# An attention-with-decay kernel: the state product leaves the natural-order y and is added to the turned y

## The chip, the cores and the metric

The kernel runs on one core of one Trainium2 chip. The metric is the device time of one execution in microseconds (us). The kernel before took 431.91 us, the median of three runs (431.82 to 432.13).

## The reference

Three layers follow one another. The first is a linear attention whose state decays, for 4 batches, 8 heads, 768 positions and a head width of 48:

```python
for t in range(S):
    kt, vt, rt, wt = (k[:, :, t], v[:, :, t], r[:, :, t], w[:, :, t])
    cur = np.einsum('bhd,bhe->bhde', u[None] * kt, vt)
    y[:, :, t] = np.einsum('bhd,bhde->bhe', rt, state + cur)
    state = wt[:, :, :, None] * state + np.einsum('bhd,bhe->bhde', kt, vt)
```

Its output, 3072 tokens of 384 values, goes through `g = h * clip(h + 3, 0, 6) / 6` with `h = x @ w_in` (384 by 2048) and `g @ w_out`, and then through a soft mixture of 8 experts with 4 slots each (`phi`, `w1`, `w2`).

## The kernel before

The attention is computed in 24 units: 4 batches times 6 chunks of 128 positions, unit n being batch n % 4 of chunk n // 4. A unit handles 8 heads as 4 pairs; a pair's two heads lie on partitions 0 to 47 and 64 to 111, so an operand that holds a pair has 112 partitions. Inside a chunk the decays are running products along the positions (two scans on VectorE, L817 and L829), keys and receptances are multiplied by them on GpSimd (L1341, L1350), and then:

- `score` (L445): keys times receptances, one 128 by 128 product for each head, two heads at once on the two halves of the array's rows; VectorE masks the result (L843), ScalarE and GpSimd split it into two half-precision parts.
- `attend` (L502): y in natural order (128 positions by 384 values) in one PSUM bank, `y_ps`. For each pair one f32 product of the decayed receptances (stationary, 112 by 128) with the state of the chunks before (moving, 112 by 96, L510), then, on top of it, six f16 products of the split scores with the split values (L516 to L520, 48 columns each). Units 0 to 3 have no state and go through `attend_first`.
- `finish_y` (L862, VectorE) scales y, adds the diagonal term and writes `y_nat`; `turn_x` (L527, TensorE) transposes it in three pieces of 128 columns back into `y_ps`; ScalarE and VectorE split the turned y into the operand of the next layer (`high_x` L1152, `low_x` L877).
- `increment` (L470): keys (transposed by `turn_keys`, L454) times values, 64 and 48 rows of output at a time; VectorE adds it to the state (`add_state`, L872, two instructions); the state of unit n is decayed by GpSimd (`decay_state`, L1359).

The second layer runs through all of this. Its 96 steps (6 groups of 512 tokens, 16 steps each) are `mlp(s)`: nine f16 products of 512 columns (L544 to L546) into one of two PSUM banks, then a relu on ScalarE (L1184), a gate and a 32 by 32 transposition on VectorE (L904, L914). `mlp(s)` waits for the gate of step s - 2. Four steps belong to one unit and are called its phases. The order on each engine is written out by hand: TensorE does the scores of unit n in phase 0, the turning of unit n - 1 at the start of phase 1 ahead of `mlp(s)` (only for the first unit behind it), the keys of unit n in phase 2 ahead of `mlp(s)` and its increment behind it, and `attend(n)` behind `mlp(s)` in phase 3. From step 5 of a group on, and in the next group, `add_logits` (L579) takes four steps' gates at a time as 32-row products, and at the turn of a group `fold_logits` (L586), `natural_logits` (L591) and `gather_slots` (L611) follow; a chain of maximum, exponential and sums on VectorE and ScalarE belongs to them. Waits are on semaphores and each engine works in order.

The part behind step 96 (from about 330 us on) is the mixture of experts.

Of the kernel before, what the change touches and what calls it, by code (L numbers as in the profile page):

```python
# [6 lines left out]
ACT = mybir.ActivationFunctionType  # L7
# [4 lines left out]
P = 128  # L12
# [8 lines left out]
Y_SCALE = V_SCALE * SCORE_SCALE  # L21
# [3 lines left out]
B, H, S, D = 4, 8, 768, 48  # L25
# [3 lines left out]
PB = H // 2  # L29
# [3 lines left out]
PD = ALIGN + D  # L33
# [10 lines left out]
W_PIECES = 8  # L44
WP = KT * FF // W_PIECES
LAST_INC = UNITS - B


def build_program(nc, wT, rkT, nat_in_dram, u, u_blocks, w_in, w_outT, w_out, phi, w1, w2, out):
    with ExitStack() as ctx:  # L50
# [21 lines left out]
        r_dec = [carve(PB * P) for _ in range(2)]  # L72
# [3 lines left out]
        scores_hi, scores_lo = (t.bitcast(F16) for t in rk_prod)  # L76
        k_nat = carve(PB * PD)
        v_hi = [carve(DM // 2).bitcast(F16) for _ in range(2)]
# [4 lines left out]
        y_nat = carve(DM)  # L83
        state = [pairs(carve(PB * 2 * D), 2 * D) for _ in range(B)]
# [12 lines left out]
        ident = sb("ident", P)  # L97
# [100 lines left out]
        k_ps = ctx.enter_context(nc.psum_tensor("k_ps", [P, 512], F32))  # L198
        inc_ps = ctx.enter_context(nc.psum_tensor("inc_ps", [P, 512], F32))
        y_ps = ctx.enter_context(nc.psum_tensor("y_ps", [P, 512], F32))  # L200
# [41 lines left out]
        decayed = sem("decayed")  # L242
# [6 lines left out]
        k_nat_done = sem("k_nat_done")  # L249
        inc_ready = sem("inc_ready")  # L250
        y_ready = sem("y_ready")
# [14 lines left out]
        x_turned = sem("x_turned")  # L266
# [65 lines left out]
        def is_unit(n):  # L332
            return 0 <= n < UNITS
# [99 lines left out]
        def _(pe):  # L433
# [66 lines left out]
                last.then_inc(y_ready, 1)  # L500

            def attend(n):  # L502
                b = n % B
                pe.wait_ge(x_lo_done, n)
                pe.wait_ge(decayed, n - B + 1)
                pe.wait_ge(v_lo_done, n - B + 1)
                pe.wait_ge(scores_lo_done, n - B + 1)
                for p in range(PB):
                    both = y_ps[:, p * 2 * D:(p + 1) * 2 * D]
                    pe.matmul(both, r_dec[n % 2][0:PD, p * P:(p + 1) * P], state[b][0:PD, p, :],  # L510
                              start=True, stop=False, skip_group_check=True)
                    for j in range(2):
                        c = both[:, j * D:(j + 1) * D]
                        here = slice((j * PB + p) * P, (j * PB + p + 1) * P)
                        there = slice((2 * p + j) * D, (2 * p + j + 1) * D)
                        pe.matmul(c, scores_hi[:, here], v_hi[n % 2][:, there], start=False, stop=False,  # L516
                                  skip_group_check=True)
                        pe.matmul(c, scores_hi[:, here], v_lo[n % 2][:, there], start=False, stop=False,
                                  skip_group_check=True)
                        last = pe.matmul(c, scores_lo[:, here], v_hi[n % 2][:, there], start=False, stop=True,  # L520
                                         skip_group_check=True)
                last.then_inc(y_ready, 1)

            def turn_x(n):
                pe.wait_ge(y_done, n + 1)
                for q in range(KT):
                    last = pe.transpose(y_ps[:, q * P:(q + 1) * P], y_nat[:, q * P:(q + 1) * P], ident[:])  # L527
                last.then_inc(x_turned, 1)

            def mlp(s):  # L530
                g, i = divmod(s, FT)
# [112 lines left out]
            for s in range(END):  # L644
                n, phase = unit_of(s)
# [164 lines left out]
        def _(dve):  # L810
# [29 lines left out]
            def mask_scores(n):  # L840
                dve.wait_ge(scores_ready, 2 * n + 2)
                dve.wait_ge(scores_lo_done, n - B)
                nc.vector.tensor_tensor(scores.rearrange("p (o n) -> p o n", o=PB),  # L843
                                        sc_ps[:, :].rearrange("p (o n) -> p o n", o=PB),
                                        mask[:].rearrange("p (o n) -> p o n", o=1).broadcast_to([P, PB, 2 * P]),
                                        ALU.mult).then_inc(masked, 2)
# [18 lines left out]

            def add_state(n):
                dve.wait_ge(inc_ready, 2 * n + 2)
                for j in range(2):
                    rows = slice(ALIGN * j, ALIGN * j + D)
                    s = state[n % B][rows, :, j * D:(j + 1) * D]  # L870
                    new = pairs(inc_ps[rows, 0:PB * 2 * D], 2 * D)[:, :, j * D:(j + 1) * D]
                    last = nc.vector.tensor_tensor(s, s, new, ALU.add)  # L872
                last.then_inc(state_added, 1)
# [137 lines left out]
            for s in range(END):  # L1011
                n, phase = unit_of(s)
                g, i = divmod(s, FT)
                if s <= 1:
                    gate(s)
                    turn_gated(s)
                if phase == 0:
                    if is_unit(n - 1):
                        finish_y(n - 1)
                    if n - 1 < LAST_INC:  # L1020
                        add_state(n - 1)
                if phase == 1:
                    if is_unit(n):
                        mask_scores(n)
                    if is_unit(n + 1):
                        scan_suffix(n + 1)
                        restart_prefix(n + 1)
                    if is_unit(n - 1) and n % B == 0 and n > B:
                        low_x(n - 1)
                    if g >= 1 and i == 2:  # L1030
                        group_maximum(g - 1)
                if phase == 2:
                    if g >= 1 and i == 3:
                        turn_weight(g - 1)
                        sum_weight(g - 1)
                    if is_unit(n - 1) and n % B:
                        low_x(n - 1)
                    if is_unit(n):
                        sum_diag(n)
                        low_v(n)  # L1040
                if s == 0:
                    low_w(1)
                    sum_diag(B)
                if phase == 3:
                    if is_unit(n + 1):
                        scan_prefix(n + 1)
                    if s == STEPS + 4:
                        dve.wait_ge(run_sum_done, C)
                        nc.vector.tensor_scalar(run_sum, run_sum, 1e-9, None, ALU.add).then_inc(sum_inv_step, 1)
                        dve.wait_ge(sum_inv_step, 1)  # L1050
                        nc.vector.reciprocal(run_sum, run_sum).then_inc(sum_inv_step, 1)
                        dve.wait_ge(sum_inv_step, 2)
                        nc.vector.tensor_scalar(fold_inv[:], fold32, run_sum, None, ALU.mult).then_inc(fold_inv_done, 1)
                        dve.wait_ge(fold_inv_done, 1)
                        nc.vector.tensor_scalar(fold_alpha, fold_inv[:], alpha, None, ALU.mult).then_inc(fold_inv_done, 1)
                    if 1 <= g < C and i == 4:
                        add_slots(g - 1)
                if s == 4:
                    dve.wait_ge(w_phi_ready, 4)
                    nc.vector.transpose(w_phi[:], l_ps[:]).then_inc(w_phi_done, 1)  # L1060
                if s == STEPS - 12:
                    cols, tiles = c_parts[0]
                    dve.wait_ge(logits_done, C - 1)
                    nc.vector.tensor_reduce(cmax[:, tiles], by_slot(soft[:, cols]), AX_X, ALU.max).then_inc(c_max_done, 1)
                if s == STEPS - 8:
                    c_inverse(0)
                if s == STEPS:
                    copy_cT(1)
                    copy_cT(0)
                if 1 < s < STEPS:  # L1070
                    gate(s)
                    turn_gated(s)
# [46 lines left out]
        def _(act):  # L1119
# [22 lines left out]
            def copy_keys(n):  # L1142
                act.wait_ge(k_turned, n + 1)
                if n:
                    act.wait_ge(inc_ready, 2 * n)
                nc.scalar.activation(k_nat, k_ps[:, 0:PB * PD], ACT.Copy, scale=Y_SCALE).then_inc(k_nat_done, 1)

            def high_x(n):
                act.wait_ge(x_turned, n + 1)
# [87 lines left out]
            for s in range(END):  # L1237
                n, phase = unit_of(s)
# [57 lines left out]
        def _(pool):  # L1296
# [46 lines left out]
            def decay_receptance(n):  # L1343
                pool.wait_ge(prefix_done, n + 1)
                pool.wait_ge(rk_rows_in[n % B], 16 * (n // B + 1))
                if n >= 2:
                    pool.wait_ge(scores_ready, 2 * (n - 1))
                    pool.wait_ge(y_ready, n - 1)
                dst, receptance, decay = receptance_of(n)
                nc.gpsimd.tensor_tensor(dst, receptance, decay, ALU.mult).then_inc(r_dec_done, 1)  # L1350

# [135 lines left out]
```

## Time and profile before

| | |
|---|---|
| median of three runs | 431.91 us |
| the profiled execution's own time | 432.12 us |
| its span, first to last instruction | 430.4 us |
| TensorE busy | 410.6 us, 95% |
| VectorE busy | 333.8 us, 78% |
| ScalarE, GpSimd busy | 155.4 us, 196.4 us |
| mean granted TensorE clock | 0.992 of 2.4 GHz |

The profile is of one execution. A share of busy time is a mean over the whole span, so it says which engine to look at and not what a change is worth. Ends of matmuls are modelled and successive matmuls overlap, so what one matmul costs is read from the distance between starts, not from its own length. An f32 product shows as two records with the same line, an f16 product as one.

### The profile page before, as it was taken

The numbers are of one execution on the slowest core, as the hardware profiler recorded it, in microseconds if no ns is written. First come the engines' busy times: TensorE is split into PE (matmuls) and PEld (weight loads), VectorE is DVE, ScalarE is ACT, GpSimd is POOL, SyncE is SP. The second block draws the span as 40 slices with busy tenths as digits, with TensorE's granted clock in tenths as the row PEclk, the third lists the DMA queues.
The fourth block names the chain that finished last, engine by engine and source line by source line (L and its number), as shares of the span: only waits on it lengthen the run. The fifth ranks groups of instructions, "written<-read, shape, count | busy, mean of one in ns | idle before, by whom it ended". The sixth has DMA issues, their size and how long they took to land.

```text
span 430.4 us, 9672 instructions
## 1 busy us (share of the span) xinstructions
PE 410.6 (95%) x3898; PEld 222.6 (52%) x3898; DVE 333.8 (78%) x535; ACT 155.4 (36%) x263; POOL 196.4 (46%) x183
## 2 busy tenths in 40 slices
PE   8999899999999999999999999989999999999981
PEld 3875555556555555555565555455554443433430
DVE  7798799998988989889889889898866687641142
ACT  2265355533334244144342342432333234211142
POOL 7747888874645663455654456634630012010000
PEclk9999999999999999999999999999999999999996
DMA  8996312468034223403440332131008961589829
GB/s 248 354 392 250 121 60 63 121 244 283 17 111 121 72 55 116 123 0 121 121 121 2 121 119 86 44 113 56 2 0 339 404 216 70 225 319 423 354 83 357
DMA packets 15245, 69.35 MB, mean 161 GB/s; under 512 B 2016, under 2 KB 2656, under 8 KB 13152
## 3 DMA queue, kind: packets, MB, share of 16 engines
q1 hardware_dynamic: 15200, 68.73, 45.0%
q8 instruction: 31, 0.51, 0.5%
q14 instruction: 14, 0.11, 0.1%
HBM read 64.00 MB, written 4.72 MB: 160 GB/s over the span
## 4 chain that ended last, share of the span: by engine, by line
PE 74%; DVE 8%; issue 6%; DMA 5%; POOL 3%; ACT 2%; SPq 0%; POOLq 0%; DVEq 0%
PE hid L544 13%; PE hid L546 12%; PE hid L545 12%; PE l_ps L579 5%; PE y_ps L510 5%; PE l_ps L611 4%; PE sc_ps L445 4%; DMA att<-rkT_dram 3%; PE hid L757 2%; PE inc_ps L470 2%; PE y_ps L527 2%; DVE att L817 2%; PE sc_ps L611 1%; PE hid L738 1%; PE sc_ps L738 1%
## 5 line engine op out<-in xcount | busy, mean ns | idle before, releaser
L1184 ACT ACTIVATE relu<-hid,three 128x512 f32<-128x512 f32 x96 | 65.9, 687 | 141.7 <-PE hid L546 140.9
L544 PE MATMUL hid<-x_split,w_split 128*128 128x512 f16 x288 | 109.4, 380 | 0.0
L546 PE MATMUL hid<-x_split,w_split 128*128 128x512 f16 x288 | 109.1, 379 | 0.0
L545 PE MATMUL hid<-x_split,w_split 128*128 128x512 f16 x288 | 109.1, 379 | 0.0
L904 DVE SCALAR_TENSOR_TENSOR gated<-relu,hid 128x512 f32<-128x512 f32 x96 | 65.1, 679 | 28.3 <-ACT relu L1184 27.7
L914 DVE STREAM_TRANSPOSE ring<-gated 128x512 f32<-128x512 f32 x96 | 68.3, 711 | 3.3
L1332 POOL TENSOR_TENSOR att<-att 128x1024 f16<-128x1024 f32 x20 | 40.5, 2026 | 50.6 <-ACT att L1129 50.6
L1350 POOL TENSOR_TENSOR att<-att 112x512 f32<-112x512 f32 x19 | 22.4, 1181 | 58.7 <-DVE att L829 58.7
L544 PEld LDWEIGHTS hid<-x_split,w_split 128*128 128x128 f16 x288 | 28.2, 98 | 37.5 <-issue 8.6
L546 PEld LDWEIGHTS hid<-x_split,w_split 128*128 128x128 f16 x288 | 28.1, 98 | 34.0
L545 PEld LDWEIGHTS hid<-x_split,w_split 128*128 128x128 f16 x288 | 28.2, 98 | 25.1 <-issue 0.3
L510 PE MATMUL y_ps<-att 112*128 112x96 f32 x160 | 33.7, 295 | 1.1 <-DVE att L888 1.1
L1341 POOL TENSOR_TENSOR att<-att 112x512 f32<-112x512 f32 x22 | 27.9, 1266 | 8.2 <-DVE att L817 6.5
L445 PEld LDWEIGHTS sc_ps<-att 48*128 48x128 f32 x384 | 23.4, 187 | 12.6 <-issue 11.8
L817 DVE TENSOR_TENSOR_SCAN att<-att 112x517 f32<-112x517 f32 x22 | 28.1, 1278 | 1.5 <-DMA att<-wT_dram 1.5
L445 PE MATMUL sc_ps<-att 48*128 48x128 f32 x384 | 27.9, 284 | 1.4 <-issue 1.1
L510 PEld LDWEIGHTS y_ps<-att 112*128 112x128 f32 x160 | 24.9, 189 | 5.5 <-issue 3.7
L611 PE MATMUL l_ps<-ring,soft 32*32 32x512 f32 x192 | 25.5, 594 | 1.8 <-DVE soft L936 1.8
L1152 ACT ACTIVATE x_split<-y_ps 128x384 f16<-128x384 f32 x24 | 11.8, 490 | 42.8 <-PE y_ps L527 42.8
L829 DVE TENSOR_TENSOR_SCAN att<-att 112x517 f32<-112x517 f32 x22 | 27.2, 1235 | 0.0
L611 PE MATMUL sc_ps<-ring,soft 32*32 32x512 f32 x384 | 26.1, 598 | 0.0
L579 PE MATMUL l_ps<-gated,w_phi 128*32 128x512 f32 x192 | 25.6, 605 | 0.4 <-DVE gated L904 0.4
(228 smaller groups left out, 752.5 us busy)
## 6 DMA issues: line engine op xcount, KB each, us to landing
att<-nat_dram SPq DMA_DIRECT2D x20, 576.0 KB, 4.1
att<-rkT_dram SPq DMA_DIRECT2D x22, 448.0 KB, 5.5
att<-w_dram SPq DMA_DIRECT2D x5, 1536.0 KB, 14.2
att<-wT_dram SPq DMA_DIRECT2D x22, 226.2 KB, 4.8
out_dram<-w_split SPq DMA_DIRECT2D x12, 384.0 KB, 3.9
stage<-w_in_dram SPq DMA_DIRECT2D x2, 1536.0 KB, 13.5
ring<-w_outT_dram SPq DMA_DIRECT2D x1, 3072.0 KB, 15.7
stage<-w_dram SPq DMA_DIRECT2D x2, 1536.0 KB, 9.9
```

The lines of the kernel that those rows point to most:

```text
L445: last = pe.matmul(sc_bank[j][:, cols], k_dec[n % 2][rows, cols], r_dec[n % 2][rows, cols], start=True, stop=True)
L510: pe.matmul(both, r_dec[n % 2][0:PD, p * P:(p + 1) * P], state[b][0:PD, p, :], start=True, stop=False, skip_group_check=True)
L544: pe.matmul(hid[s % 2][:], high, x_high, start=(q == 0), stop=False)
L545: pe.matmul(hid[s % 2][:], high, x_low, start=False, stop=False)
L546: last = pe.matmul(hid[s % 2][:], low, x_high, start=False, stop=(q == KT - 1))
L579: pe.matmul(l_ps[SLOTS * c:SLOTS * (c + 1), :], w_phi[:, i * SLOTS:(i + 1) * SLOTS], gated_tile(g * FT + i), start=(m == 0), stop=(m == 3) ...
L611: ins = pe.matmul(dg_bank[a][SLOTS * c:SLOTS * (c + 1), :], weight_T[SLOTS * a:SLOTS * (a + 1), b * SLOTS:(b + 1) * SLOTS], ring_group(g, ...
L817: nc.vector.tensor_tensor_scan(suffix[0:PD, ::-1], w_rows_of(n)[0:PD, ::-1], mark[0:PD, ::-1], 1.0, ALU.mult, ALU.add).then_inc(suffix_don ...
L904: nc.vector.scalar_tensor_tensor(gated_tile(s), relu_tile(s), 6.0 * GATE, hid[s % 2][:], ALU.min, ALU.mult).then_inc(gated_done, 1)
L914: nc.vector.transpose(ring_tile(s), gated_tile(s)).then_inc(gated_turned, 1)
L1184: nc.scalar.activation(relu_tile(s), hid[s % 2][:], ACT.Relu, bias=three[:], scale=GATE / H_SCALE)\
L1332: nc.gpsimd.tensor_tensor(scores_lo, scores, scores_hi, ALU.subtract).then_inc(scores_lo_done, 1)
```

## The change

The state product leaves `attend`, whose first score product now starts the accumulation. In `turn_x` the three transpositions put the turned y into `y_ps`, and eight f32 products are then added on top of it in the same bank: the state is the stationary operand, 64 or 32 of its 96 columns at a time, and the receptances of a pair stream as 128 columns. The eight pieces are cut so that each lies in one 128-row block of the turned y and starts at a multiple of its own height. Both operations are part of the same signal `x_turned`.

What follows from it elsewhere: the state is not scaled any more, so `copy_keys` loses its scale; `add_state(n)` also waits for the turned y of unit n and moves from phase 0 of VectorE to phase 1, behind the mask (for unit 4 to phase 2); the receptances of unit n wait for the turned y of unit n - 2 where they waited for its natural y; `attend` does not wait for the decayed state, the product in `turn_x` does.

```diff
+STATE_ROWS = ((0, 64), (64, 32), (96, 32), (128, 64), (192, 64), (256, 32), (288, 32), (320, 64))
...
             def attend(n):
-                b = n % B
                 pe.wait_ge(x_lo_done, n)
-                pe.wait_ge(decayed, n - B + 1)
                 pe.wait_ge(v_lo_done, n - B + 1)
                 pe.wait_ge(scores_lo_done, n - B + 1)
                 for p in range(PB):
                     both = y_ps[:, p * 2 * D:(p + 1) * 2 * D]
-                    pe.matmul(both, r_dec[n % 2][0:PD, p * P:(p + 1) * P], state[b][0:PD, p, :],
-                              start=True, stop=False, skip_group_check=True)
...
             def turn_x(n):
                 pe.wait_ge(y_done, n + 1)
                 for q in range(KT):
-                    last = pe.transpose(y_ps[:, q * P:(q + 1) * P], y_nat[:, q * P:(q + 1) * P], ident[:])
+                    last = pe.matmul(y_ps[:, q * P:(q + 1) * P], y_nat[:, q * P:(q + 1) * P], ident[:], start=(q == 0),
+                                     stop=True, is_transpose=True, skip_group_check=True)
+                if n >= B:
+                    last = add_state_product(n)
                 last.then_inc(x_turned, 1)
+
+            def add_state_product(n):
+                pe.wait_ge(decayed, n - B + 1)
+                for first, size in STATE_ROWS:
+                    q, row = divmod(first, P)
+                    p, col = divmod(first, 2 * D)
+                    last = pe.matmul(y_ps[row:row + size, q * P:(q + 1) * P], state[n % B][0:PD, p, col:col + size],
+                                     r_dec[n % 2][0:PD, p * P:(p + 1) * P], start=False, stop=True,
+                                     skip_group_check=True)
+                return last
...
             def add_state(n):
                 dve.wait_ge(inc_ready, 2 * n + 2)
+                dve.wait_ge(x_turned, n + 1)
...
                 if phase == 0:
                     if is_unit(n - 1):
                         finish_y(n - 1)
-                    if n - 1 < LAST_INC:
-                        add_state(n - 1)
                 if phase == 1:
                     if is_unit(n):
                         mask_scores(n)
+                    if B < n - 1 < LAST_INC:
+                        add_state(n - 1)
...
                 if phase == 2:
+                    if n == B + 1:
+                        add_state(B)
...
-                nc.scalar.activation(k_nat, k_ps[:, 0:PB * PD], ACT.Copy, scale=Y_SCALE).then_inc(k_nat_done, 1)
+                nc.scalar.activation(k_nat, k_ps[:, 0:PB * PD], ACT.Copy).then_inc(k_nat_done, 1)
...
-                    pool.wait_ge(y_ready, n - 1)
+                    pool.wait_ge(x_turned, n - 1)
```

On TensorE, around the turning of unit 8 at the end of the first group (L445 are scores, L527 the transpositions, L544 to L546 an `mlp` step), the order before is:

```order
L586 MATMUL l_ps<-soft,fold 128x512
L445 MATMUL sc_ps<-att 128x128 x8
L527 MATMUL y_ps<-ident,att 128x128 x3
L544 MATMUL hid<-x_split,w_split 128x512
L545 MATMUL hid<-x_split,w_split 128x512
L546 MATMUL hid<-x_split,w_split 128x512
```

In the changed kernel the same place reads as follows (L524 are the transpositions, L535 the state products, L554 to L556 the `mlp` step):

```order
L596 MATMUL l_ps<-soft,fold 128x512
L446 MATMUL sc_ps<-att 128x128 x8
L524 MATMUL y_ps<-ident,att 128x128 x3
L535 MATMUL y_ps<-att 64x128
L535 MATMUL y_ps<-att 32x128 x2
L535 MATMUL y_ps<-att 64x128 x2
L535 MATMUL y_ps<-att 32x128 x2
L535 MATMUL y_ps<-att 64x128
L554 MATMUL hid<-x_split,w_split 128x512
```

Eight products with 64, 32, 32, 64, 64, 32, 32 and 64 rows of output now stand between the last transposition and the `mlp` step; the four products of 96 columns are gone from `attend`, which stands one `mlp` step ahead of these rows.

On VectorE, in the same two phases, the order before is (L862 finishes y, L872 adds to the state, L904 and L914 are gate and transposition, L843 is the mask, L817 and L822 begin the next unit's decays, L921 is the group's maximum):

```order
L862 SCALAR_TENSOR_TENSOR att<-y_ps,att 128x384
L872 TENSOR_TENSOR att<-att,inc_ps 48x4x48 x2
L904 SCALAR_TENSOR_TENSOR gated<-relu,hid 128x512
L914 STREAM_TRANSPOSE ring<-gated 128x512
L843 TENSOR_TENSOR att<-sc_ps,mask 128x1024
L817 SCALAR_TENSOR_TENSOR att<-att 112x517
L822 RECIPROCAL att<-att 112x4
L921 TENSOR_REDUCE stats<-l_ps 128x1
```

And in the changed kernel (L872, L883, L915, L925, L853, L827, L832 and L932 are the same instructions):

```order
L872 SCALAR_TENSOR_TENSOR att<-y_ps,att 128x384
L915 SCALAR_TENSOR_TENSOR gated<-relu,hid 128x512
L925 STREAM_TRANSPOSE ring<-gated 128x512
L853 TENSOR_TENSOR att<-sc_ps,mask 128x1024
L883 TENSOR_TENSOR att<-att,inc_ps 48x4x48 x2
L827 SCALAR_TENSOR_TENSOR att<-att 112x517
L832 RECIPROCAL att<-att 112x4
L932 TENSOR_REDUCE stats<-l_ps 128x1
```

The two additions to the state have moved from ahead of a gate to between the mask and the scan.

## Rows read from the trace of the kernel before

**Rows 1.** The page: TensorE's share, granted clock by slices, last chain.

```profile
PE 410.6 (95%) x3898; PEld 222.6 (52%) x3898; DVE 333.8 (78%) x535; ACT 155.4 (36%) x263; POOL 196.4 (46%) x183
...
PEclk9999999999999999999999999999999999999996
...
PE 74%; DVE 8%; issue 6%; DMA 5%; POOL 3%; ACT 2%; SPq 0%; POOLq 0%; DVEq 0%
```

**Rows 2.** Groups by line, TensorE: shapes, count | busy us, mean ns | idle before.

```profile
L510 PE MATMUL y_ps<-att 112*128 112x96 f32 x160 | 33.7, 295 | 1.1 <-DVE att L888 1.1
```

**Rows 3.** Timeline of TensorE, one `attend`: start us, length us, instruction, count.

```profile
189.28 0.38 PE L546 MATMUL hid<-x_split,w_split 128*128 128x512 f16 x1
189.49 0.36 PE L510 MATMUL y_ps<-att 112*128 112x96 f32 x2
189.69 0.19 PE L516 MATMUL y_ps<-att 128*128 128x48 f16 x1
...
189.82 0.18 PE L520 MATMUL y_ps<-att 128*128 128x48 f16 x1
189.84 0.44 PE L510 MATMUL y_ps<-att 112*128 112x96 f32 x2
...
191.14 0.38 PE L544 MATMUL hid<-x_split,w_split 128*128 128x512 f16 x1
```

**Rows 4.** Timeline of TensorE, one `increment`: whole, its third and its last record.

```profile
186.63 0.38 PE L546 MATMUL hid<-x_split,w_split 128*128 128x512 f16 x1
186.94 0.67 PE L470 MATMUL inc_ps<-att 128*64 128x48 f32 x16
...
187.04 0.22 PE L470 MATMUL inc_ps<-att 128*64 128x48 f32 x1
...
187.39 0.22 PE L470 MATMUL inc_ps<-att 128*64 128x48 f32 x1
187.54 0.39 PE L544 MATMUL hid<-x_split,w_split 128*128 128x512 f16 x1
```

**Rows 5.** Timeline of TensorE: scores, logits, turning, with single records inside.

```profile
193.18 1.16 PE L445 MATMUL sc_ps<-att 48*128 48x128 f32 x16
...
193.39 0.27 PE L445 MATMUL sc_ps<-att 48*128 48x128 f32 x1
...
194.07 0.27 PE L445 MATMUL sc_ps<-att 48*128 48x128 f32 x1
194.27 0.64 PE L579 MATMUL l_ps<-gated,w_phi 128*32 128x512 f32 x4
...
194.72 0.61 PE L579 MATMUL l_ps<-gated,w_phi 128*32 128x512 f32 x4
195.26 0.55 PE L527 MATMUL y_ps<-ident,att 128*128 128x128 f32 x3
195.65 0.38 PE L544 MATMUL hid<-x_split,w_split 128*128 128x512 f16 x1
```

**Rows 6.** Timeline at the turn of a group, VectorE, and TensorE's next `mlp` step.

```profile
160.21 0.71 DVE L872 TENSOR_TENSOR att<-att,inc_ps 48x192 f32<-48x192 f32 x2
162.00 0.69 DVE L904 SCALAR_TENSOR_TENSOR gated<-relu,hid 128x512 f32<-128x512 f32 x1 [1.08 <-ACT relu L1184]
...
163.36 1.19 DVE L843 TENSOR_TENSOR att<-sc_ps,mask 128x1024 f32<-128x1024 f32 x1
164.47 1.22 DVE L817 TENSOR_TENSOR_SCAN att<-att 112x517 f32<-112x517 f32 x1
...
163.51 0.38 PE L544 MATMUL hid<-x_split,w_split 128*128 128x512 f16 x1
```

**Rows 7.** Timeline of TensorE: three matmuls ahead of which it waited.

```profile
70.91 0.32 PE L510 MATMUL y_ps<-att 112*128 112x96 f32 x1 [0.53 <-DVE att L888]
...
169.48 0.26 PE L470 MATMUL inc_ps<-att 128*64 128x48 f32 x2 [0.69 <-ACT att L1146]
...
47.57 0.38 PE L445 MATMUL sc_ps<-att 48*128 48x128 f32 x2 [1.08 <-issue]
```

More of the change, by code:

```diff
@@ L515, in attend @@
                         there = slice((2 * p + j) * D, (2 * p + j + 1) * D)
-                        pe.matmul(c, scores_hi[:, here], v_hi[n % 2][:, there], start=False, stop=False,
+                        pe.matmul(c, scores_hi[:, here], v_hi[n % 2][:, there], start=True, stop=False,
                                   skip_group_check=True)
```

## Prediction

> **What bounds the kernel now.** I began with the page. TensorE is busy for 410.6 of 430.4 us and makes up 74% of the chain that ended last; the granted clock stands in its upper tenth in every slice but the last [rows 1]. A busy TensorE can still have slack, so the second view was its timeline over one unit. There the matmuls follow each other start to start without a hole: after the last `mlp` matmul at 189.28 the first of `attend` starts at 189.49, the same 0.21 us that one `mlp` matmul of 512 columns takes [rows 3]. The third view was where TensorE did wait. It waits in few places: ahead of `attend` for the low half of the values (0.53 us in unit 6, the same again in unit 7), at three turns of a group for the chain behind the group's maximum (0.69 us ahead of the increment in the row shown), and once, at 47.57, ahead of the scores of unit 5 (1.08 us) [rows 7]. So up to the end of the units the time is the sum of TensorE's spacings, and what the change adds or takes between two starts passes into the total, apart from these few places.
>
> **What goes.** Units 4 to 23, which are 20, have a state product: 160 records of L510 are 20 units by 4 pairs by 2 [rows 2]. One `attend` takes 1.65 us, from its first start at 189.49 to the next `mlp` step at 191.14 [rows 3]. Six score products of a pair lie between 189.69 and 189.84, which is 0.155 us for six or 0.026 each, so the 24 that remain take 0.62 us. The change takes 1.65 - 0.62 = 1.03 us out of a unit. In unit 4 that gives nothing: the scores of unit 5 stand behind it and wait 1.08 us anyway [rows 7], for receptances that GpSimd is still decaying. So 19 x 1.03 = 19.6 us.
>
> **What comes.** Sixteen records (eight f32 products) behind the transpositions. The trace has no product of this kind, so I build it from three prices.
>
> First, the stream. The scores are f32 with 128 moving columns as well: from 193.39 to 194.07 six records of one half of the array start, 0.11 us apart, while the other half runs beside them [rows 5]. Two records of a product on one place of the array therefore take 0.22 us. Products on different columns of the array do run at the same time: the four 32-column products of the logits all start at 194.27 and their second records at 194.72, 0.45 us later, although each streams 512 columns [rows 5]. Were there no such overlap, the eight would take 8 x 0.22 = 1.76 us; with perfect overlap the three that share a place take 0.66.
>
> Second, the first load of weights, which nothing hides: in the increment the second record of a place comes 0.10 us after the first and the rest every 0.06 ((187.39 - 187.04) / 6) [rows 4], so 0.04 more for 64 columns; for 32 columns it is 0.45 - 0.43 = 0.02 [rows 5].
>
> Third, the price of a change of shape. Wherever two neighbours use the array with different tile shapes, the next start is late: 186.63 to 186.94 is 0.31 where 0.21 is the stream (full array to 64 columns); 187.39 to 187.54 is 0.15 where 0.06 is (64 columns to full); 194.07 to 194.27 is 0.20 where 0.11 is (half rows to 32 columns); 194.72 to 195.26 is 0.54 where 0.43 is (32 columns to full) [rows 4, 5]. That is 0.09 to 0.11 each time, whatever the pair; I take 0.095. Where the shape stays (112 rows of 128 columns behind an `mlp` matmul, the transpositions ahead of one) nothing is added [rows 3, 5].
>
> The sequence is 64 | 32 32 | 64 64 | 32 32 | 64 rows of output: five stretches, with four changes of height inside and one at either end. What no row shows is a change between 64 and 32 columns. Its price lies between nothing, if pieces on different columns don't care about each other's height, and 0.095 us with all of the stretch before it drained. I take 0.095, since every change of shape that the trace has costs that, also the ones in which the number of rows stays at 128 and only the columns change. Then a 64-row stretch takes 0.22 + 0.04 = 0.26, a 32-row stretch 0.24, and the block 3 x 0.26 + 2 x 0.24 + 6 x 0.095 = 1.83 us. 20 units give 36.6 us.
>
> The Trainium skill speaks on both sides here. "TensorEngine Tiling (Array Packing)", Performance Considerations, recommends just this swap with column tiles where the moving operand is narrow, with up to a twofold gain; its Key Properties say that a change of the tiling mode, as opposed to a change of tile, drains the engine, and list 128 by 64 and 128 by 32 as two modes. By the second rule the sum above stands; by the first alone the block would be 0.89 us. The trace agrees with the drain on every pair it has (0.09 to 0.11 us); the pair 64 and 32 no row shows.
>
> **What the waits give back.** The waits of units 6 and 7 stand behind a chain on VectorE. It now holds the two additions to the state as well (0.71 us [rows 6]), but TensorE arrives 1.83 us later, so both waits of 0.53 us [rows 7] go: -1.1 us. At the three turns VectorE's chain from the mask to the exponential sets the wait for the keys. Before, the scan began at 164.47, 0.96 us after the `mlp` step at 163.51 [rows 6]. Now VectorE waits for the turned y, which comes at about the start of that step, adds 0.71 and scans some 0.8 behind it: 0.1 us earlier relative to TensorE, -0.3 us over the three. In phase 0 the additions lay in front of a gate that had 1.08 us of idle time [rows 6], so taking them away there gives nothing. In phase 1 their cover is the longer turning itself. GpSimd's new wait is for a turning two units back, and ScalarE's copy without a scale is the same instruction; both cost nothing. ScalarE's split of the turned y and of the scores comes later by as much as TensorE does, and `attend` is two steps away.
>
> **Sum.** +36.6 - 19.6 - 1.1 - 0.3 = +15.6 us on the profiled execution's 432.12 us, which is 447.7. The runs' median lies 0.2 below that execution: 447.5 us. With the three prices moved by their rounding (0.08 to 0.11 for a change, 0.02 to 0.06 for a first load) this case alone gives 444 to 451.
>
> **Rivals.**
>
> Free heights, on the other side: a 32-row piece starts while a 64-row piece on other columns runs, and nothing drains inside the block. What speaks for it is that the increments' 64 and 48 columns run side by side and even overtake each other; against it, that both sit in tiles of the same height. Then the places work as queues of three products: 0.04 + 6 x 0.11 + 2 x 0.095 = 0.89 us, 17.8 for 20 units, against 19.6 gone and some 0.6 less waiting: -2.4, or 429.5 us. It decides for faster from a block below about 1.0 us.
>
> A drain by place only: a piece waits for the pieces of another height on its own columns, not for all. Each column then sees one change inside: 0.04 + 0.44 + 0.095 + 0.02 + 0.22 + 0.19 = 1.01 us, 20.2 in all, less 19.6 and 0.6: nothing, or 431.9 us, no change. For it: array columns are served separately. Against it: the same drains.
>
> The wait on VectorE takes over: with a short block the mask (1.19 us) ends after the turning, the additions are no longer covered and push the chain at three turns and in units 6 and 7 by 0.71 us: up to +3.6 on the case of free heights, 433.1. Against it: the mask starts at 163.36 and ends 0.15 us behind the step's start even then.
>
> No overlap inside a stretch: 8 x 0.25 + 0.57 = 2.57 us, 51.4 for 20 units, less 19.6 and 1.4: 462 us. The logits' rows speak against it.
>
> **Chances.** Drain at each change of height 0.70, free heights 0.16, drain by place 0.08, VectorE 0.04, no overlap 0.02. The likeliest case gives the time, 447.5 us. The range goes from the free heights, 429, to the top of the likeliest, 451. A measurement of this kernel can tell 0.2% (0.9 us) from no change: faster 0.17, within it 0.09, slower 0.74.
>
> **What would show it.** In the profile after: from the first transposition to the next `mlp` matmul 2.2 us (0.39 before) if each change drains, 1.3 if heights are free, 1.4 if by place. Inside, the 64-row and the 32-row records start in five stretches with 0.2 us between the last start of one and the first of the next, or interleaved if they are free. `attend` takes 0.62 us. The waits ahead of `attend` in units 6 and 7 are gone. I am wrong if the 32-row products start while the first 64-row product still streams.

## The result, and the profile after

The changed kernel takes 448.71 us, the median of four runs (447.99 to 449.84), the kernel before beside it 432.02 us (431.82 to 432.14, four runs): a ratio of 1.0387, with a 95% interval of 1.0375 to 1.0399. It is slower, by 16.7 us; the forecast was 447.5 us.

The page of the changed kernel answers to [rows 1]:

```profile
PE 427.8 (96%) x4058; PEld 217.8 (49%) x4058; DVE 331.6 (74%) x535; ACT 153.9 (34%) x263; POOL 199.9 (45%) x183
...
PEclk9999899999999999999999999999999999999996
...
PE 84%; DMA 5%; DVE 4%; issue 3%; ACT 1%; POOL 1%; SPq 0%; DVEq 0%; POOLq 0%
```

TensorE is busy for 17.2 us more, its share of the last chain has grown from 74 to 84%, and one slice of the granted clock has an 8. This profile is of the run of 449.37 us.

The block in question, by the starts of its records (timeline of TensorE: start us, length us, instruction, count):

```profile
204.29 0.55 PE L524 MATMUL y_ps<-ident,att 128*128 128x128 f32 x3
...
204.77 0.43 PE L535 MATMUL y_ps<-att 112*64 112x128 f32 x2
...
204.93 0.27 PE L535 MATMUL y_ps<-att 112*64 112x128 f32 x1
...
205.13 0.41 PE L535 MATMUL y_ps<-att 112*32 112x128 f32 x4
...
205.47 0.44 PE L535 MATMUL y_ps<-att 112*64 112x128 f32 x4
...
205.84 0.41 PE L535 MATMUL y_ps<-att 112*32 112x128 f32 x4
...
206.19 0.43 PE L535 MATMUL y_ps<-att 112*64 112x128 f32 x2
206.55 0.39 PE L554 MATMUL hid<-x_split,w_split 128*128 128x512 f16 x1
```

Five stretches, 0.34 to 0.37 us apart. Within the third the two 64-row products run side by side (four records in the time of two), so the array is shared inside a stretch and not between stretches. The clearest is the second stretch: its 32-row products write rows 64 to 127, on columns of the array that the first product leaves free, and still do not start beside it. The first product's second record starts at 204.93 and the next stretch 0.20 us behind it, where 0.11 is the stream of one record [rows 5]. From the first transposition to the `mlp` step it is 2.26 us, where it was 0.39 [rows 5]: 1.87 more.

`attend` answers to [rows 3]: without the four state products it is 0.61 us long (0.61 in 15 of the 20 units, 0.70 in the others).

```profile
74.68 0.38 PE L556 MATMUL hid<-x_split,w_split 128*128 128x512 f16 x1
74.89 0.19 PE L513 MATMUL y_ps<-att 128*128 128x48 f16 x1
...
75.47 0.18 PE L517 MATMUL y_ps<-att 128*128 128x48 f16 x1
75.50 0.38 PE L554 MATMUL hid<-x_split,w_split 128*128 128x512 f16 x1
```

I gave each matmul the distance to the next start, set idle time of more than 0.15 us apart, and summed by function over both traces. That is a ledger of the whole execution; the rows that did not change are left out:

| us, TensorE | before | after | difference |
|---|---|---|---|
| the eight state products in the turning | 0.0 | 35.6 | +35.6 |
| `turn_x` itself (one change of shape more) | 9.6 | 11.4 | +1.8 |
| `attend` | 34.0 | 12.6 | -21.4 |
| `mlp` and `score`, same instructions | 217.3 | 218.9 | +1.6 |
| waits ahead of scores | 1.4 | 3.8 | +2.4 |
| waits ahead of the gathering of slots | 1.8 | 0.4 | -1.5 |
| waits ahead of `attend` | 1.1 | 0.0 | -1.1 |
| waits ahead of the increment | 1.4 | 1.6 | +0.2 |

With -0.4 for the matmuls at the very start it is +17.2 us, and the profiled execution of after took 449.37 us against 432.12, 17.25 more.

The row of `mlp` and `score` is not work but the clock: in the run below that keeps the full clock the two come to 217.3 us again. The waits that answer to [rows 7]: units 6 and 7 no longer wait ahead of `attend`, the wait at the turn of a group has gone from 0.69 to 0.43 us, but unit 5's scores wait 2.21 us where they waited 1.08, and behind that wait the granted clock falls (timeline, then two tables by stretch, after and before: start and end, its length, then busy time and count of PE, PEld (TensorE's weight loads), DVE, ACT and POOL, granted clock, DMA share, GB/s):

```profile
47.22 0.42 PE L446 MATMUL sc_ps<-att 48*128 48x128 f32 x2 [2.21 <-issue]
...
178.71 0.26 PE L471 MATMUL inc_ps<-att 128*64 128x48 f32 x2 [0.43 <-ACT att L1159]
```

```profile
44.00:47.20 3.20, 1.01 (x9) 0.11 (x9) 3.09 (x5) 0.00 (x0) 2.90 (x3) 1.00 0.14 24
47.20:49.10 1.90, 1.88 (x17) 1.68 (x18) 0.00 (x0) 0.00 (x0) 1.82 (x3) 0.56 0.78 270
49.10:51.90 2.80, 2.80 (x11) 1.15 (x11) 2.67 (x2) 0.00 (x0) 2.44 (x2) 0.69 0.79 253
```

```profile
44.00:47.50 3.50, 2.49 (x39) 1.54 (x36) 3.47 (x7) 0.06 (x1) 2.86 (x3) 1.00 0.10 19
47.50:49.10 1.60, 1.53 (x18) 1.21 (x19) 0.85 (x3) 0.00 (x0) 1.60 (x2) 1.00 0.78 276
49.10:51.90 2.80, 2.80 (x19) 1.14 (x17) 2.47 (x3) 0.76 (x2) 2.72 (x3) 1.00 0.90 270
```

TensorE was busy for 1.01 of 3.20 us, and then works 3.4 us at 1.2 instead of 2.4 GHz (a mean of 0.56 over 1.90 and of 0.69 over 2.80 us). Before, the same place was busy for 2.49 of 3.50 us and stayed at full clock. The four runs stand at 448.0, 448.1, 449.4 and 449.8 us, those below with a mean clock of 0.992, those above with 0.982 and 0.988. Only the run of 449.37 us was profiled, and the mean clock of a run does not by itself tell where it fell: the kernel before has means from 0.985 to 0.994 among runs within 0.5 us of each other.

### The profile page after: what moved, and what is told of

The parts are those of the page before. It is cut to its first block, busy times and chain, and to the rows that moved or that the text cites. A ratio compares the mean times of both kernels' runs of the same rounds, so it can differ in the third digit from the quotient of the medians.

```text
span 447.7 us, 9988 instructions
## 1 busy us (share of the span) xinstructions
PE 427.8 (96%) x4058; PEld 217.8 (49%) x4058; DVE 331.6 (74%) x535; ACT 153.9 (34%) x263; POOL 199.9 (45%) x183
## 4 chain that ended last, share of the span: by engine, by line
PE 84%; DMA 5%; DVE 4%; issue 3%; ACT 1%; POOL 1%; SPq 0%; DVEq 0%; POOLq 0%
PE hid L554 14%; PE hid L556 13%; PE hid L555 13%; PE y_ps L535 8%; PE l_ps L589 5%; PE sc_ps L446 5%; PE l_ps L621 4%; DMA att<-rkT_dram 3%; PE inc_ps L471 2%; PE hid L767 2%; PE y_ps L524 2%; PE sc_ps L621 1%; PE k_ps L455 1%; PE l_ps L596 1%; PE hid L748 1%
## 5 line engine op out<-in xcount | busy, mean ns | idle before, releaser
L554 PE MATMUL hid<-x_split,w_split 128*128 128x512 f16 x288 | 110.1, 382 | 0.0
L556 PE MATMUL hid<-x_split,w_split 128*128 128x512 f16 x288 | 109.4, 380 | 0.0
L915 DVE SCALAR_TENSOR_TENSOR gated<-relu,hid 128x512 f32<-128x512 f32 x96 | 65.0, 677 | 30.8 <-ACT relu L1197 30.8
L1345 POOL TENSOR_TENSOR att<-att 128x1024 f16<-128x1024 f32 x20 | 45.0, 2252 | 62.2 <-ACT att L1142 62.2
L925 DVE STREAM_TRANSPOSE ring<-gated 128x512 f32<-128x512 f32 x96 | 68.3, 711 | 3.3
L554 PEld LDWEIGHTS hid<-x_split,w_split 128*128 128x128 f16 x288 | 28.2, 98 | 41.0 <-issue 11.5
L556 PEld LDWEIGHTS hid<-x_split,w_split 128*128 128x128 f16 x288 | 28.2, 98 | 34.4 <-issue 0.6
L535 PE MATMUL y_ps<-att 112*64 112x128 f32 (+1 forms) x320 | 37.0, 291 | 0.0
L827 DVE TENSOR_TENSOR_SCAN att<-att 112x517 f32<-112x517 f32 x22 | 28.1, 1278 | 1.6 <-DMA att<-wT_dram 1.2
L535 PEld LDWEIGHTS y_ps<-att 112*64 112x64 f32 (+1 forms) x320 | 17.4, 121 | 18.1 <-issue 18.1
## 6 DMA issues: line engine op xcount, KB each, us to landing
att<-rkT_dram SPq DMA_DIRECT2D x22, 448.0 KB, 5.4
```

The source lines that it names most:

```text
L535: last = pe.matmul(y_ps[row:row + size, q * P:(q + 1) * P], state[n % B][0:PD, p, col:col + size], r_dec[n % 2][0:PD, p * P:(p + 1) * P], ...
L554: pe.matmul(hid[s % 2][:], high, x_high, start=(q == 0), stop=False)
L556: last = pe.matmul(hid[s % 2][:], low, x_high, start=False, stop=(q == KT - 1))
L827: nc.vector.tensor_tensor_scan(suffix[0:PD, ::-1], w_rows_of(n)[0:PD, ::-1], mark[0:PD, ::-1], 1.0, ALU.mult, ALU.add).then_inc(suffix_don ...
L915: nc.vector.scalar_tensor_tensor(gated_tile(s), relu_tile(s), 6.0 * GATE, hid[s % 2][:], ALU.min, ALU.mult).then_inc(gated_done, 1)
L925: nc.vector.transpose(ring_tile(s), gated_tile(s)).then_inc(gated_turned, 1)
```

## The experiments

**The order of the heights.** Theory A: each change of height drains the array and costs some 0.095 us plus the overlap that it breaks. Theory B: the eight products simply cost what they stream, since 8 x 0.22 = 1.76 us is close to the measured 1.78. Only the order of the pieces changes:

```diff
-STATE_ROWS = ((0, 64), (64, 32), (96, 32), (128, 64), (192, 64), (256, 32), (288, 32), (320, 64))
+STATE_ROWS = ((0, 64), (192, 64), (128, 64), (320, 64), (64, 32), (96, 32), (256, 32), (288, 32))
```

> The same eight products in another order: the four of 64 rows first (alternating between the two halves of the columns), then the four of 32 rows. Theory A (every change of height drains the array): one change inside instead of four. From the changed kernel's starts the block is 0.09 to come in, 0.16 + 3 x 0.107 + 0.10 for the 64s and 0.36 for the 32s, 1.03 us where it was 1.87: 0.84 less for each of 20 units, some 16.8 us less, about 432 us. Theory B (the eight products cost what they stream, 8 x 0.22 one after the other): no change of the block, 448 us.

Measured: 433.56 us (433.19 to 433.79, four runs; before 432.01). The block, from the first transposition to the `mlp` step, is 1.43 us, 1.04 more than the transpositions alone. That is as expected. The time is 1.5 us above the 432 expected, and TensorE's waits are longer, 12.2 us in all where the kernel before has 9.0. The block's lines:

```profile
195.82 0.55 PE L524 MATMUL y_ps<-ident,att 128*128 128x128 f32 x3
196.30 1.02 PE L535 MATMUL y_ps<-att 112*64 112x128 f32 x16
197.25 0.39 PE L554 MATMUL hid<-x_split,w_split 128*128 128x512 f16 x1
```

The other way round, with as many changes as eight pieces allow:

```diff
+STATE_ROWS = ((0, 64), (64, 32), (128, 64), (96, 32), (192, 64), (256, 32), (320, 64), (288, 32))
```

> The same eight products with the heights alternating, 64, 32, 64, 32 and so on: seven changes inside instead of four, and no two products side by side. Theory A: four stretches of 0.363 and four of 0.335 and 0.09 to come in, 2.88 us for the block where it was 1.87, 20 us more: about 468 us. Theory B: the same streams, no change, 448 us.

Measured: 470.01 us (one run).

```profile
214.77 0.55 PE L524 MATMUL y_ps<-ident,att 128*128 128x128 f32 x3
215.25 2.86 PE L535 MATMUL y_ps<-att 112*64 112x128 f32 x16
218.04 0.39 PE L554 MATMUL hid<-x_split,w_split 128*128 128x512 f16 x1
```

3.27 us, 2.88 beyond the transpositions. The same eight products cost 1.04, 1.87 or 2.88 us by their order alone, with one, four and seven changes of height inside. B has fallen. The run is 2 us above the 468 expected; 1.6 of them are the granted clock, which falls behind unit 5's wait in this profile too (0.81 from 47.2 to 49.1 us and 0.52 from there to 51.9).

**One height.** Twelve products of 32 rows, 50% more of them, and no change inside.

```diff
+STATE_ROWS = tuple((32 * i, 32) for i in range(12))
```

> Twelve products of 32 rows instead of eight of 64 and 32, so no change of height inside the block at all; four columns of the array, three products on each. Theory A (drain at each change of height): 0.09 + 0.13 + 5 x 0.107 + 0.12 = 0.88 us for the block where it was 1.87, 20 us less: about 428 us, and that is less than the kernel before, since the block then costs less than the 1.04 us which attend lost. Theory B (the products cost what they stream, one after the other): twelve times 0.22, 2.6 us for the block, 15 us more, 464 us.

```profile
195.05 0.87 PE L535 MATMUL y_ps<-att 112*32 112x128 f32 x24
195.85 0.39 PE L554 MATMUL hid<-x_split,w_split 128*128 128x512 f16 x1
```

The block is 0.80 us from its first start to the `mlp` step and with the change of shape ahead of it 0.89, as expected. The time is not: 434.21 us (430.5 to 438.67, twelve runs; before 432.01), where I had 428. Two things are in it. TensorE now waits 5.6 us ahead of scores (1.4 before), and the runs spread over 8 us; the profiled one of them (433.02 us) stops for 1.7 us in the middle of the last gathering of slots, in front of an instruction that the profile shows waiting for nothing:

```profile
381.30 0.62 PE L621 MATMUL k_ps<-ring,soft 32*32 32x512 f32 x3 [1.71 <-issue]
```

**No state product.** The eight products are left out, so units 4 to 23 lack what the earlier chunks contribute; everything else is the changed kernel.

```diff
-                if n >= B:
-                    last = add_state_product(n)
```

> The state product is left out altogether (units 4 to 23 get no contribution of earlier chunks); all else is the changed kernel. Theory A (the time up to the last unit is the sum of TensorE's spacings): the block of 1.87 us goes 20 times, 37.5 us less, 411 us, plus what TensorE then waits. Theory C (VectorE's chain, with the additions to the state now between mask and scan, becomes the bound where the longer turning no longer covers it): waits of up to 0.7 us at several units and turns of a group, 414 us or more.

Measured: 422.06 us (one run), not 411. The products do go from TensorE (37.4 us), and 11 us come back as waits: 9.1 us ahead of scores (3.8 in the changed kernel), 3.7 ahead of increments (1.6), 2.2 ahead of the gathering (0.4), 1.2 ahead of `attend` and 0.7 ahead of `mlp`. The timeline at one of them:

```profile
141.46 1.19 DVE L837 TENSOR_TENSOR_SCAN att<-att 112x517 f32<-112x517 f32 x1
...
142.73 1.18 POOL L1361 TENSOR_TENSOR att<-att 112x512 f32<-112x512 f32 x1 [2.96 <-DVE att L837]
...
144.01 0.38 PE L446 MATMUL sc_ps<-att 48*128 48x128 f32 x2 [0.74 <-issue]
```

VectorE's second scan ends at 142.65, GpSimd decays the receptances until 143.91, and the scores start 0.1 us later. Theory A for this run holds for the work and not for the time: some 10 us below the kernel before, the chain of scan, receptances and scores is what TensorE waits for most, ahead of ten units' scores. C named VectorE's chain and 414 us or more, and the chain does begin at VectorE's scan; whether the additions to the state are what makes the scan late, no run shows.

**The clock at unit 5.** Six matmuls without use go into the longer wait.

```diff
                         attend(B)
                         weigh_phi(1)
+                        pe.wait_ge(masked, 2 * n)
+                        stay_warm(6, sc_bank[0])
```

> The changed kernel, and six f16 matmuls of 512 columns without use in the 2.2 us that TensorE waits for the receptances of unit 5, behind the waits for the masks and ahead of that for the receptances. Theory D (where the changed kernel takes 449.4 to 449.8 us and not 448.0, the granted clock fell after this longer wait): every run near 448.0 us, and the profile shows the full clock from 47 to 52 us. Rival (the spread comes from somewhere else, the weights' transfers or the code): the runs keep both times.

Measured: 448.17 us (447.8 to 448.5, four runs). The same stretches as above:

```profile
44.00:47.20 3.20, 2.47 (x18) 0.66 (x14) 3.15 (x5) 0.00 (x0) 2.85 (x3) 1.00 0.16 22
47.20:49.10 1.90, 1.83 (x20) 1.38 (x21) 0.56 (x1) 0.00 (x0) 1.82 (x3) 1.00 0.76 265
49.10:51.90 2.80, 2.80 (x22) 1.43 (x22) 2.17 (x3) 0.00 (x0) 2.80 (x2) 1.00 0.86 259
```

The clock stays full, `mlp` and `score` take 217.3 us again instead of 218.9, and no run comes near 449.4. So the fall of the clock cost the profiled run of the changed kernel 1.6 us. That the run of 449.84 had the same fall fits, but it was not profiled.

**Twelve products and the six matmuls.**

> The twelve products of 32 rows, and the six matmuls in the wait ahead of the scores of unit 5. Theory D: the runs above 430.5 us go for the part that is the clock at unit 5, the median at 431 us or below. Rival (the spread of 430.5 to 438.7 us comes from the stop of 1.7 us inside the last gathering of slots and the like, late in the kernel): it stays, median 434 us.

Measured: 433.21 us (430.5 to 436.33, twelve runs). Four runs stand at 430.5 to 430.8, eight at 433 to 436. So the clock at unit 5 was not what spreads this kernel; the rival stands. The profile of the twelve products alone agrees: its scores of unit 5 waited 2.21 us, and the granted clock stayed at 1.00 from 40 to 52 us.

**The scan moved.** In addition VectorE's second scan goes from the start of phase 3 to the end of phase 2.

```diff
+                if phase == 2 and is_unit(n + 1) or s == 0:
+                    scan_prefix(n + 1)
                 if phase == 3:
-                    if is_unit(n + 1):
-                        scan_prefix(n + 1)
```

> As the run before, and VectorE's second scan (of the decays for the receptances of the next unit) moved from the start of phase 3 to the end of phase 2, ahead of a gate for which ScalarE is still at work. Theory E (what the shorter attention does not give back is waited ahead of the scores, for the receptances that GpSimd decays after this scan): the waits ahead of the scores of units 6, 7 and 23 (0.86, 0.83 and 0.94 us) go, 2 to 2.5 us less than without the move. Rival (the scores wait for the keys or for the masks, or VectorE's gates come later by as much): no change or slower.

Measured: 433.29 us (432.91 to 437.45, twelve runs); its fastest run is 2.4 us above the fastest without the move. The waits ahead of scores did go, from 4.2 to 0.8 us, so theory E has the chain right (the units are 7, 8 and 23; the expectation counts the first two one too low). But the gates come later and `mlp` waits 3.9 us, which was nothing before, as the rival has it. Ahead of the scores of unit 7 without the move, and ahead of an `mlp` step of unit 6 with it:

```profile
74.95 0.38 PE L446 MATMUL sc_ps<-att 48*128 48x128 f32 x2 [0.84 <-issue]
```

```profile
74.22 0.39 PE L554 MATMUL hid<-x_split,w_split 128*128 128x512 f16 x1 [1.07 <-DVE gated L917]
```

> The kernel before with the same move of the scan and nothing else. Theory E: its scores wait in one place only (unit 5), which the move does not touch, so no change, 432 us, within 0.5 us.

Measured: 432.77 us (432.56 to 433.21, ten runs; before 432.03), a ratio of 1.0012 with an interval of 0.9993 to 1.0031. The medians are 0.7 us apart, outside the 0.5 us that I expected, and all ten runs lie above all but two of the 29 of before, one of which stood at 436.72 us and widens the interval. Here too `mlp` gets a wait (1.6 us in all) that it did not have, while the 1.1 us ahead of `attend` go.

**Where the code's pieces end.** The profile's queue of instructions moves packets of 16 KB, 33 of them in the run with twelve products (31 before); I take them for TensorE's code, since their number goes with its matmuls (31 at 3898, 34 at 4294). In the run that stopped, one of them was fetched at 378.9 us, 3.8 us after the last gathering's first matmul; in the profiled run with the six matmuls, which did not stop, the same one was fetched 0.3 us ahead of it. To move the ends of the pieces without other work, the first ten matmuls without use are cut smaller (40 of 128 columns, then 80 of 64):

```diff
-            keep_awake(10)
+            keep_awake(40, 128)
```

> As the twelve products of 32 rows with the six matmuls in unit 5's wait, and TensorE's first ten matmuls without use (512 columns, ahead of the first scores) cut into forty of 128 columns: the same streaming, some 60 instructions more. Theory F (half of the runs of the kernel with twelve products stand at 433 to 436 us and not at 430.5 because a piece of TensorE's code is fetched late inside the last gathering of slots, as the profile of its first version shows with a stop of 1.7 us; with the code moved by 60 instructions the end of a piece falls elsewhere): another share of slow runs, at best all near 430.5 us. Rival (the spread does not hang on the code's place): as before, 430.5 to 436 us with a median of 433.

> The same with eighty matmuls of 64 columns, some 140 instructions more. Theory F: again another share of slow runs, the ends of the pieces having moved by more than half a piece; at best all near 430.5 us. Rival: as before, median 433 us.

Measured: 430.93 us (430.49 to 435.11, eleven runs) and 430.72 us (430.32 to 433.64, twelve runs), with the kernel before at 431.89. One of eleven and three of twelve runs lie above 432, where it was eight of twelve. In the profiles of both no fetch falls into the gathering: the next stands 0.2 and 0.6 us behind the start of its last matmul. So the counts and the fetches fit theory F, but they do not prove it: both versions ran on another chip than the one with eight of twelve, and the version without the cut was not run there. That the chip makes the difference is a rival that no run here excludes. Nor is it shown that a late piece of code is the stop in each of the higher runs, since only one of them was profiled. The second of the two is the fastest version here: a ratio of 0.9985 to the kernel before, with an interval of 0.9971 to 0.9999, so 0.15% at the best estimate.

## Why the prediction was right

The step on which it stood, that a change between 64 and 32 columns costs what every other change of tile shape in the trace costs, held: the block costs 1.87 us a unit against 1.83 in the sum, and three orders of the same pieces follow the count of changes. Of its rivals, free heights and a drain by place fell with the starts of the second stretch, and the missing overlap with the third. The wait on VectorE was priced for a short block, and where the block was short (twelve products) it did not come as described: the waits at two turns were 0.45 us, below the 0.69 of the kernel before, and what grew were the waits for receptances ahead of scores. The rule of the Trainium skill on this ("TensorEngine Tiling (Array Packing)", Key Properties: a change of mode drains, a change of tile does not) agrees with every pair of shapes seen here, 64 and 32 columns now among them at 0.09 to 0.10 us (0.20 from the last start of a stretch to the next, less the 0.11 of the stream); what the traces show is this late start, not what the array does in it. The advice of the Trainium skill, in the same page's Performance Considerations, to swap the operands and use column tiles is given for 64 moving columns or fewer; `attend` moved 96. For this product the swap clearly saves TensorE time only with tiles of one width, 0.89 us for the block against 1.04 us saved in `attend`, and even so the medians of twelve runs were 434.2 and 433.2 us, not below the kernel before.

What `attend` loses was 1.03 us in the sum and is 1.04 in the rows shown, 1.07 as a mean of the 20 units. That unit 5's scores would eat the gain of unit 4 was right (their wait grew by 1.13 us). The waits of units 6 and 7 went as expected (-1.1). The sum's two large terms, +36.6 and -19.6, came out at +37.4 and -20.3 (with unit 5's wait).

Three terms were off, and partly cancelled. The turns of a group gave back 2.0 us (0.26 at two of them, 1.46 ahead of one gathering) where I had 0.3: I had compared only the start of VectorE's scan with TensorE's step, and the third of the three waits, 1.64 us, stood ahead of a gathering and not of an increment. Waits that I had at nothing came to 2.0 us: 0.75 ahead of the increment of unit 5, 0.17 and 0.16 ahead of two units' scores, and 0.94 ahead of the last unit's.

The first of these comes from the change itself. The increment of unit 5 waits for the addition of unit 4's to the state, which had moved to phase 2 and now ends just ahead of it (VectorE, then TensorE):

```profile
57.60 0.68 DVE L883 TENSOR_TENSOR att<-att,inc_ps 48x192 f32<-48x192 f32 x2
...
58.38 0.25 PE L471 MATMUL inc_ps<-att 128*64 128x48 f32 x2 [0.75 <-issue]
```

The last unit's scores wait for the receptances that GpSimd decays behind VectorE's scan. As I read the order, the shorter `attend` brings the scores there too early, since no keys and no increment stand between:

```profile
323.19 1.18 POOL L1363 TENSOR_TENSOR att<-att 112x512 f32<-112x512 f32 x1 [3.46 <-DVE att L839]
...
324.46 0.38 PE L446 MATMUL sc_ps<-att 48*128 48x128 f32 x2 [0.94 <-issue]
```

And I had costed the wait at unit 5 at its length alone; in the profiled execution the clock that fell behind it is the 1.6 us by which `mlp` and `score` grew. The runs at 448.0 us stand 0.5 above the forecast of 447.5. That it came so close is in part luck: the turns (-1.7 against the sum) and the waits (+2.0) nearly cancel.

## What to carry to other kernels

When small products are packed into the array, count the changes of tile shape in the order in which they are issued, and price each from two rows of the trace: the distance across the change less the distance without it. Group pieces of one shape, or cut all of them to the smaller one, even if that makes more of them (1.04 and 0.89 us here, against 1.87 mixed). And a gain on a busy engine stops where the next chain stands: leaving the work out altogether, as in the run without the state product, shows how far away that is (10 us below the kernel before here, not 21).

## What the runs showed that was not expected

A wait of TensorE that grew from 1.08 to 2.21 us cost more than itself: in the profiled run the granted clock fell to 0.56 and 0.69 in the next two stretches, 1.6 us on top. Six matmuls without use in the wait kept it at 1.00. The fall does not come each time: of the five profiles with this wait of 2.2 us two show it (the changed kernel and the alternating heights) and three do not (two heights, twelve products, no state product).

The kernel with twelve products, whose work on TensorE is 3.2 us shorter than before's, had runs of 430.5 and of 432.4 to 438.7 us. With TensorE's first ten matmuls without use cut into 80, on another chip, nine of twelve runs stood at 430.3 to 431.6. Runs of before stayed within 0.7 us in that comparison; beside the runs with the six matmuls one of 29 stood at 436.72 us, so a rare long run is not this kernel's alone.
